# Which PSUM banks carry the last tile of block 0 and the first of block 1, and the order in which ScalarE serves the first four tiles

## The reference, cut to what matters

```
x = attn(x, weight)                  # causal mix of 7 tokens with softmax weights, per head; (2, 4096, 192)
x = x.reshape(8192, 192)
h1 = sigmoid(x @ moe_w_gate) * (x @ moe_w_val)       # 192 -> 1536, then
y  = h1 @ moe_w_out                                  # 1536 -> 192
h  = y @ moe2_w_in                                   # 192 -> 2048
g  = where(h > 0, h, exp(min(h, 0)) - 1)
z  = g @ moe2_w_out                                  # 2048 -> 192
```

## Time and profile before

| | us |
|---|---|
| median of 3 executions | 1189.92 |
| the three | 1189.92, 1189.48, 1190.04 |
| the profiled execution, its time | 1187.65 |
| the profiled execution, its span | 1185.9 |
| PE busy | 1172.3 |
| DVE busy | 917.9 |
| ACT busy | 630.2 |
| POOL busy | 83.8 |

### The profile page before, as it was taken

How to read it: one execution, slowest core, us unless ns; L and a number is a source line. 1 busy time by engine, 2 the same in 40 slices (tenths; PEclk the granted TensorE clock), 3 DMA queues, 4 the chain that set the end, 5 groups by cost and what they waited for, 6 DMA issues and landing times.

```text
span 1185.9 us, 27165 instructions
## 1 busy us (share of the span) xinstructions
PE 1172.3 (99%) x10228; PEld 1058.5 (89%) x10228; DVE 917.9 (77%) x1495; ACT 630.2 (53%) x1097; POOL 83.8 (7%) x87
## 2 busy tenths in 40 slices
PE   7899999999999999999999999999999999999998
PEld 5788889998899999999998888888889999998897
DVE  7588777787777877778777787777877777787786
ACT  7456555455554645545455454554645545465554
POOL 4181001010010100101000010100101001010000
PEclk9999999999999999999999999999999999999999
DMA  6021101011010010100101001110001101001000
GB/s 209 20 72 37 32 18 34 19 32 31 18 35 31 18 31 18 35 31 18 31 18 49 18 18 31 30 36 18 22 27 36 31 18 35 31 18 31 10 11 27
DMA packets 14023, 38.05 MB, mean 32 GB/s; under 512 B 2224, under 2 KB 2224, under 8 KB 14000
## 3 DMA queue, kind: packets, MB, share of 16 engines
q1 hardware_dynamic: 13776, 37.60, 11.0%
q10 hardware_dynamic: 224, 0.14, 0.1%
HBM read 15.71 MB, written 6.29 MB: 19 GB/s over the span
## 4 chain that ended last, share of the span: by engine, by line
PE 96%; DVE 2%; ACT 1%; issue 1%; DMA 0%; DVEq 0%; ACTq 0%
PE hid L263 53%; PE z_acc_a L281 14%; PE y_acc_a L281 11%; PE z_acc_b L281 9%; PE y_acc_b L281 7%; PE z_acc_a L336 1%; DVE hid L755 1%; PE y_acc_a L263 0%; DVE y_acc_a L679 0%; DMA cw<-conv_w 0%; DVE y_acc_b L679 0%; ACT h_split L531 0%; ACT curve L526 0%; DVE h_split L717 0%; ACT xs L545 0%
## 5 line engine op out<-in xcount | busy, mean ns | idle before, releaser
L263 PE MATMUL hid<-xs,gw 64*128 64x512 f32 x3240 | 606.4, 386 | 0.0
L263 PEld LDWEIGHTS hid<-xs,gw 64*128 64x128 f32 x3240 | 504.2, 184 | 32.5 <-DVE h_split L717 0.6
L263 PE MATMUL hid<-ys,ew 64*128 64x512 f32 x2160 | 478.8, 387 | 0.0
L531 ACT CAST h_split<-hidden 128x512 fp32r<-128x512 f32 x437 | 270.0, 618 | 271.6 <-DVE hidden L755 230.1
L263 PEld LDWEIGHTS hid<-ys,ew 64*128 64x128 f32 x2160 | 377.7, 184 | 24.6 <-DVE h_split L717 0.5
L526 ACT ACTIVATE curve<-hid 128x512 f32<-128x512 f32 x446 | 263.3, 597 | 256.3 <-PE hid L263 256.1
L281 PE MATMUL z_acc_a<-h_split,ew 64*128 64x512 f32 x1440 | 365.3, 387 | 0.0
L717 DVE TENSOR_TENSOR h_split<-hidden,h_split 128x512 fp32r<-128x512 f32 x437 | 306.6, 702 | 32.8 <-ACT h_split L531 27.7
L281 PE MATMUL y_acc_a<-h_split,gw 64*128 64x512 f32 x1080 | 302.9, 387 | 0.0
L281 PEld LDWEIGHTS z_acc_a<-h_split,ew 64*128 64x128 f32 x1440 | 265.1, 184 | 16.9
L281 PE MATMUL z_acc_b<-h_split,ew 64*128 64x512 f32 x960 | 256.3, 387 | 0.0
(11 more groups left out here) (92 smaller groups left out, 494.3 us busy)
## 6 DMA issues: line engine op xcount, KB each, us to landing
x_in<-x_windows SPq DMA_DIRECT2D x16, 518.0 KB, 3.3
ys<-ys SPq DMA_DIRECT2D x30, 256.0 KB, 3.6
xs<-xs SPq DMA_DIRECT2D x30, 256.0 KB, 3.4
out<-z_out SPq DMA_DIRECT2D x16, 256.0 KB, 2.0
raw_g<-g_weights SPq DMA_DIRECT2D x12, 288.0 KB, 4.8
raw_e<-e_weights SPq DMA_DIRECT2D x8, 384.0 KB, 4.1
out<-z_out SPq DMA_DIRECT2D x15, 128.0 KB, 2.3
x_in<-x_windows SPq DMA_DIRECT2D x1, 259.0 KB, 2.8
```

The costliest lines, as they stand in the source:

```text
L263: return nc.tensor.matmul(acc[:], w[rows, at:at + P], inp[rows, features], start=s == 0, stop=s == last)
L531: nc.scalar.copy(h_split[:, t % RING, 0], hidden_at(base, t)).then_inc(hi_done, 1)
```

## The change

`gate_val` now takes `prev`. In block 0 only tile 2 uses `y_acc`; tile 11 uses `hid[0:2]`. In block 1 (`prev == "G"`) tile 0 uses `y_acc`; its other tiles and all later blocks keep the pairs of `hid`. The wait of slot 11 for `x_ready` 4 is taken out; the one at the start of block 1 was there before and stays.

ACT casts the weights of tile 5 ahead of the first curve too. For tiles 0 to 3 of block 0 its order becomes: curve 0; curve 1, high 0; curve 2, high 1, weights 6; curve 3, high 2, weights 7, high 3. From tile 4 on it is: curve t, weights t + 4, high t. DVE's order becomes: hidden 0; hidden 1, low 0; hidden 2, low 1; hidden 3, low 2, low 3, third tap. Then follow two taps a tile in tiles 4 to 8 and the last tap in tile 9, ahead of its low part. Both halves of `split_x(1, 1)` now stand ahead of the curve and of the hidden product of tile 10. POOL waits for the first low part of a hidden tile before it begins with the weights of tile 5.

```diff
-        def gate_val(n_is_first, t):
-
-            if n_is_first and t in (2, NG - 1):
+        def gate_val(prev, t):
+
+
+            if t == {None: 2, "G": 0}.get(prev):
                 return y_acc
-            at = 2 * ((t + 1) % 2 if n_is_first and t > 2 else t % 2)
+            at = 2 * ((t + 1) % 2 if prev is None and t > 2 else t % 2)
             return hid[at:at + 2]
...
-                    if prev is None and t == NG - 1:
-                        pe.wait_ge(x_ready, 4)
-                    gate, val = gate_val(prev is None, t)
+                    gate, val = gate_val(prev, t)
...
-                    bend(base, t, ACT.Sigmoid, gate_val(prev is None, t)[0])
+                    if prev is None and t == 10:
+                        split_x(1, 1)
+                    bend(base, t, ACT.Sigmoid, gate_val(prev, t)[0])
                     if prev == "E" and t == 0:
                         take_y(base - NE, y_acc)
-                    if prev is None and t + AHEAD < NG:
-                        split_g_weights(t + AHEAD)
+                    if prev is None and t < 4:
+
+                        if t:
+                            hi_part(base, t - 1)
+                        if t > 1:
+                            split_g_weights(t + AHEAD - 1)
+                        if t == 3:
+                            hi_part(base, t)
+                        continue
+                    if prev is None and t + AHEAD - 1 < NG:
+                        split_g_weights(t + AHEAD - 1)
                     hi_part(base, t)
...
-                    if prev is None and t == 9:
-                        split_x(1, 1)
...
-            for t in range(3, AHEAD):
+            for t in range(3, AHEAD + 1):
                 split_g_weights(t)
...
+                    if prev is None and t == 10:
+                        split_x(1, 1, xs)
                     dve.wait_ge(curve_done, base + t + 1)
...
-                    m = 2 * (t - {None: 2, "G": 5, "E": 3}[prev])
-                    if (0 if prev else EARLY) <= m < 2 * K:
+                    if prev is None and t < 4:
+                        if t:
+                            lo_part(base, t - 1)
+                        if t == 3:
+                            lo_part(base, t)
+                            tap(1, EARLY)
+                        continue
+                    m = 2 * t - 5 if prev is None else 2 * (t - {"G": 5, "E": 3}[prev])
+                    if 0 <= m < 2 * K:
                         tap(n + 1, m)
                     lo_part(base, t)
-                    if (0 if prev else EARLY) <= m < 2 * K:
+                    if 0 <= m + 1 < 2 * K:
                         tap(n + 1, m + 1)
                     if prev is None and t == 7:
                         split_x(1, 0, xs)
-                    if prev is None and t == 10:
-                        split_x(1, 1, xs)
...
             split_g_last_columns(0)
+
+            pool.wait_ge(lo_done, 1)
             for t in range(BY_DVE, NG):
                 split_g_weights(t)
```

More of the change, by code:

```diff
@@ L183, in hidden_at @@
             in_bank = isinstance(base, int) and base == 0 and t > 0
-            return gate_val(True, t)[1][:] if in_bank else hidden[:, t % RING]
+            return gate_val(None, t)[1][:] if in_bank else hidden[:, t % RING]
         block = ctx.enter_context(nc.Block())
@@ L346, in both @@
                     last = 4 if t == 0 else 8
-                    gate, val = gate_val(True, t)
+                    gate, val = gate_val(None, t)
                     lower = hid_mm(LOW, gate, gw[:, t], inp, s, last)
@@ L751, in g_phase @@
                         lo_part(base, -1)
+                    if prev is None and t == 10:
+                        split_x(1, 1, xs)
                     dve.wait_ge(curve_done, base + t + 1)
                     dve.wait_ge(val_done, n * NG + t + 1)
-                    val = gate_val(prev is None, t)[1]
+                    val = gate_val(prev, t)[1]
                     nc.vector.tensor_tensor(hidden_at(base, t), val[:], curve[:, t % 2],
```

## The result

The changed kernel takes 1182.18 us (median of 4 executions, 1181.78 to 1182.55) where the kernel before takes 1189.70 us (median of 4, 1188.52 to 1190.04): a ratio of 0.9938, with a 95% interval of 0.9921 to 0.9956. The forecast was 1182.6. In the profiled execution (1181.78 us) the span is 1180.1 us instead of 1185.9. Lines of code have moved by a few: L263, L281, L704, L717, L755, L855 are L264, L282, L712, L725, L765, L870 in the changed kernel.

What follows compares the result with a forecast made beforehand. PE was taken as the bound, busy 1172.3 of 1185.9 us, with 7.82 us lost before block 1. Gains of 2.05 + 0.20 + 5.03 = 7.28 us gave 1182.6 us; 8 in 10 for 1181.7 to 1184.2.

Steps and rivals of the forecast that it cites:

- Tiles 0 to 3: Start of block 0: with the new orders slots 4 and 5 lose nothing, 2.05 us won.
- The clash of the third tap: DVE's third tap, due at 22.40 us beside POOL's weights of tile 7: taken as 1.4 us, bounds 0.74 and 1.74.
- POOL behind low 0: POOL starts tile 5's weights at 18.9 instead of 17.04 us: no price, and low 0 no longer lengthened (1.07 against 0.69).
- Slot 10: PE's slot 10 in block 0, start 38.71 us, due 38.49: 0.22 us lost where 0.42 was, 0.20 won.
- The pause and the clock: Around slot 11: the 3.51 us pause before it and the 1.52 us of lower clock behind go, 5.03 us won.
- Block 1 in `y_acc`: Start of block 1: low part of the split ends at 43.20 us, block 1 due at 45.37, 2.17 us to spare.
- The span: Span of the profiled execution: from 1185.9 to 1178.6 us.
- a longer DVE chain: Rival: DVE is late by more than its spare 0.29 us, which stands before slot 10; 1183.3 to 1184 us, chance 0.08.
- a wait that moves: Rival: slot 11 passes but block 1 stands before `x_ready` 4, lower clock behind; up to 1187.7 us, chance 0.04.
- a lower clock elsewhere: Rival: one slot elsewhere runs at the lower clock, costing 1.5 us; 1184.1 us, chance 0.03.
- the late landing of tile 5's raw weights: Rival "slower": raw tile lands after 15.1 us, delaying curve 0 and slot 3; 1192.2 us at 25 us, chance 0.02.
- the 0.5 us that the prediction weighed for it: First tap of the second group on DVE, blocked by POOL some 0.5 us at about 30 us; sum unchanged either way.

Runs made afterwards that it cites:

- the exchange run: Changed kernel with ACT's second exchange of the first group one tile later, behind high 8 instead of high 7: 1184.04 us, again 1183.88 us.
- The banks alone: Kernel before with only the new choice of banks and no wait of slot 11 for `x_ready` 4, every order as before: 1186.38 us, ratio 0.9955.
- the orders alone: Changed kernel with the banks of before (tile 11 in `y_acc` behind its wait, tile 0 of block 1 in `hid`): 1185.56 us.
- the memsets: Changed kernel with 3, 7 or 10 extra DVE memsets ahead of DVE's half of `split_x(1, 1)`: 1180.70, 1188.61 and 1187.11 us.

## Why the prediction was right, step by step

- *Tiles 0 to 3* (2.05 us). Right, at 2.01 us (slot 3 to slot 6 took 27.86 - 17.43 = 10.43 and takes 25.67 - 17.25 = 8.42): slots 4 to 6 follow each other in 3.18 and 3.19 us, where slots 4 and 5 were 0.73 and 1.19 too long and slot 4 was 0.13 late. Hidden 3 ends 3.6 us after the start of slot 3, as worked out (20.99 - 17.43 = 3.56, measured 20.84 - 17.25 = 3.59).
- *The clash of the third tap.* Worked out at 1.4 us, measured 1.42. The eight other traces in which it meets POOL at this place have 1.13 to 1.42: it depends on how far POOL's operation has got when the tap starts.
- *POOL behind low 0.* Right that it costs nothing, wrong in what it is good for. I gave it 0.4 us of low 0; the run without it shows low 0 free of any clash, and 1.24 us lost on two earlier operations, because the early cast has moved POOL's start and the inputs landed late. The step that failed is the one that looked at POOL's timing of before instead of the new one.
- *Slot 10* (0.20 us). The chain is right: hidden 8 starts at 37.91 and slot 10 at 38.72 (38.71), and the exchange run shows that this chain is all of the stall. The hundredths are luck, and the term is too large. Slot 6 started 0.14 us earlier than forecast (25.67 against 25.81), but the chain on DVE and ACT from hidden 6 on did not (29.16 against 29.18). So from slot 6 to slot 10 it takes 13.05 us where it took 13.10, 0.05 us won.
- *The pause and the clock* (5.03 us). Right in both parts: from slot 10 to block 1 it took 52.65 - 40.96 = 11.69 us and takes 45.36 - 38.72 = 6.64, 5.05 less, at granted clock 1.00. The banks alone and the orders alone each leave 0.2 to 1.05 us of pause at full clock, and the memsets bring back pause and clock, 1.7 us for the clock (with 7 of them the stretch from slot 4 to the first DMA of `ys`, 71.93 - 19.88 = 52.05 us, is 4.15 longer than the 67.20 - 19.30 = 47.90 of the changed kernel, and 2.47 of this lie before block 1).
- *Block 1 in `y_acc`.* Split at 43.22 (43.20), block 1 at 45.36 (45.37). The closeness of the last number, and of the total, has luck in it: the gain at block 1 is 2.01 + 0.05 + 5.05 and 0.18 from an opening that ended earlier, which the prediction did not have, together 7.29 against 7.28. The 0.18 is within what the opening differs by between executions of one kernel (last section), and it covers the 0.15 missing at slot 10.
- *The rest of the kernel* was to move with it. It did: at the first DMA of `ys`, issued during block 1, the gain is 7.30 us (74.50 against 67.20, last section). From the start of block 1 to there it takes 21.84 us, and 21.85 before, so no new wait of PE appears.
- *The span* came out at 1180.1, not 1178.6. That is no lost gain: the profiled execution of before was one with a quick loop. The second trace of the changed kernel has a loop of the same pace as that one, and a span of 1178.3.

- *The median* of 1182.18 against 1182.6 has luck in it too: the forecast took the profiled execution as 2.27 us below the median, as before, and in the changed kernel it is 0.40 below.

Of the prediction's rivals, a longer DVE chain, a wait that moves and a lower clock elsewhere did not occur in the changed kernel; the late landing of tile 5's raw weights did not either (the three casts run from 13.80 to 15.62 without a gap).

## What to carry to other kernels

A pause of the bounding engine is worth reading from both ends: what the waiting step needs the resource for (here two banks for one tile), and who else could use it at that time. Giving the contested banks to the next tile that waits for the same event anyway took 4.8 us out with no work made faster; the orders alone, which give the event earlier, took out 5.7, of which 3.8 are the same pause and clock, so such gains must be worked out together, not added. And when one engine gets its input earlier, work out again what its new time collides with: an early cast let POOL start on top of DVE, which cost 1.25 us in the one trace without the added wait, an execution with a late landing.

## What the runs showed of the hardware that I had not expected

**The clock falls after less than I thought.** The granted clock stayed at 1.00 over pauses of PE of 1.05 us, and went to 0.50 (1.2 GHz) for some 3 us after pauses of 2.36, 3.5 and 4.4 us. Each of these lengths but 3.5 was seen in one trace only, and none between 1.05 and 2.36 was made. In the second trace of the kernel before, the fall came about 1 us after PE had started again.

**The loop has more than one pace at full clock.** The timeline of SP shows the first DMA of `ys` for block 0, just ahead of the loop, and the second one for block 14, at its end; in the kernel before, its second trace, the changed kernel and its second trace, one fence for each kernel:

```profile
74.50 0.53 SPq L212 DMA_DIRECT2D ys<-ys  x1
...
1076.69 0.60 SPq L213 DMA_DIRECT2D ys<-ys  x1
```

```profile
74.55 0.53 SPq L212 DMA_DIRECT2D ys<-ys  x1
...
1079.93 0.60 SPq L213 DMA_DIRECT2D ys<-ys  x1
```

```profile
67.20 0.53 SPq L213 DMA_DIRECT2D ys<-ys  x1
...
1070.67 0.60 SPq L214 DMA_DIRECT2D ys<-ys  x1
```

```profile
66.98 0.53 SPq L213 DMA_DIRECT2D ys<-ys  x1
...
1069.03 0.60 SPq L214 DMA_DIRECT2D ys<-ys  x1
```

The same work takes 1002.2, 1005.4, 1003.5 and 1002.1 us. Over all fourteen traces it is 1002.0 to 1002.5 or 1005.3 to 1005.5, once 1003.5, whatever the kernel. That is 0.3%, as much as half of the gain studied here. What sets it stays open; no run here was made for it.

**The opening differs between executions.** The load of block 1's inputs, issued at 9.6 to 9.7 us, landed 3.3 to 5.3 us later. DVE's first tap of block 1 started between 13.4 and 15.0 us (in the thirteen traces where it stands ahead of the tiles), and in the four where it came after 14.2 us slot 3 of PE waited 0.58 to 1.69 us for hidden 0, since the taps stand ahead of it on DVE; the 1.69 includes the 1.25 us of the run without POOL's wait. The landing isn't all of it: the eight matmuls of PE's first stretch, which start at 5.0 to 5.2 us, were busy for 5.13 to 6.68 us, and in the three traces with over 6.5 us slot 3 started at 17.8 to 18.0 without any such wait. Why they differ stays open.

**DVE and POOL.** An operation of DVE with both inputs in SBUF that starts while one of POOL's is under way ended about 0.55 us after POOL's (25.05 against 24.49 us before, 23.70 against 23.15 in the changed kernel), and here even `tensor_scalar` with one tensor from SBUF and its result in SBUF was lengthened, from 0.49 to 1.13 us. The Trainium skill, SBUF — State Buffer, section "Who interferes with whom", lists both kinds as ones that can be blocked, `tensor_scalar` only if its operands meet conditions that the prediction left out, and the traces agree. With its result in PSUM `tensor_scalar` took 0.74 us at 29.77 us in the changed kernel, with POOL at work from 29.16 to 30.45, and 0.74 us at 30.77 in the kernel before, with POOL idle until 31.34. So the 0.5 us that the prediction weighed for it do not arise.
